# Behind the attention loop of a fused attention, Fourier mixing and MLP kernel: three engines' orders rearranged (updates in a row on POOL, weight roundings moved on ACT, the second chunk's row statistics moved on DVE)

## The reference, cut to what matters

```python
mask = q_bucket[:, :, :, None] == k_bucket[:, :, None, :]
scores = np.where(mask, scale * np.matmul(q, k.transpose(0, 1, 3, 2)), -1e9)
attn = softmax(scores)                   # 2 batches, 8 heads, 768 x 768
x = attn @ v                             # heads side by side: 2 x 768 x 512
...
X = np.fft.fft(np.fft.fft(x, axis=1), axis=2)
u = x + np.real(X)
un = (u - mean(u)) / np.sqrt(var(u) + 1e-06)        # over each row of 512
x = u + np.maximum(un @ w_ch1, 0.0) @ w_ch2         # 512 -> 2048 -> 512
...
theta = x @ w_theta
u = x + w_tok_r @ (x * cos(theta)) + w_tok_i @ (x * sin(theta))
out = u + np.maximum(u @ w_ch, 0.0)
```

## Time and profile before

| | us |
|---|---|
| median of 3 runs (780.46 to 783.19) | 782.68 |
| the profiled execution's own time | 781.82 |
| its span in the trace | 779.5 |
| PE busy | 732.8 (94%) |
| DVE busy | 438.5 (56%) |
| ACT busy | 333.8 (43%) |
| POOL busy | 298.7 (38%) |

### The profile page before, as it was taken

One profiled execution on the slowest core, in us unless ns is written; L12 is line 12 of the kernel. 1 busy time (PEld: TensorE's weight loads), 2 busy tenths in 40 slices (PEclk: granted clock), 3 DMA queues, 4 the chain that ended last, 5 costly groups with the idle time before them and its releaser, 6 DMA issues.

```text
span 779.5 us, 11008 instructions
## 1 busy us (share of the span) xinstructions
PE 732.8 (94%) x3826; PEld 615.4 (79%) x3826; DVE 438.5 (56%) x755; ACT 333.8 (43%) x693; POOL 298.7 (38%) x274
## 2 busy tenths in 40 slices
PE   3999999999998996899999999999977999999998
PEld 2788988988887775788888888888865787888876
DVE  2999999999999556623221121211146657754533
ACT  2889989988888334233101111101114333322201
POOL 3788887788784257545000000200002124312100
PEclk9999999999999997999999999999998999999999
DMA  6366644334320104322000003100012220000002
GB/s 170 96 151 149 165 103 117 95 90 116 76 72 15 42 1 135 89 74 68 1 0 1 1 1 98 51 1 0 1 55 77 62 92 27 1 14 27 14 28 81
DMA packets 48135, 47.86 MB, mean 61 GB/s; under 512 B 15828, under 2 KB 35924, under 8 KB 48084
## 3 DMA queue, kind: packets, MB, share of 16 engines
q1 hardware_dynamic: 44244, 41.65, 19.8%
q0 software_dynamic: 3840, 5.53, 2.7%
HBM read 30.26 MB, written 3.15 MB: 43 GB/s over the span
## 4 chain that ended last, share of the span: by engine, by line
PE 71%; DVE 16%; issue 5%; POOL 2%; ACT 2%; DMA 2%; SPq 1%; POOLq 0%; ACTq 0%; DVEq 0%
PE PS L908 19%; PE PS L910 19%; PE PS L909 19%; DVE negmax L1259 6%; DVE ETL L1269 4%; DVE affine L1262 2%; PE PS L999 2%; PE PS L1039 2%; PE PS L1025 2%; PE PS L1024 2%; PE PS L1040 2%; PE PS L1137 1%; PE PS L1144 1%; ACT OS L811 1%; ACT E L799 1%
## 5 line engine op out<-in xcount | busy, mean ns | idle before, releaser
L1369 DVE SCALAR_TENSOR_TENSOR HL<-PS,HH 128x512 fp32r<-128x512 f32 x48 | 33.1, 690 | 176.5 <-ACT HH L869 176.5
L869 ACT ACTIVATE HH<-PS 128x512 fp32r<-128x512 f32 x48 | 28.7, 598 | 200.2 <-PE PS L910 200.2
L799 ACT ACTIVATE E<-PS,affine 128x768 f32<-128x768 f32 x96 | 95.2, 991 | 38.3 <-DVE affine L1262 36.1
L1259 DVE TENSOR_REDUCE negmax<-PS 128x1 f32<-128x768 f32 x96 | 90.8, 945 | 16.7 <-PE PS L1025 15.5
L1269 DVE TENSOR_TENSOR ETL<-PS,ETH 128x384 fp32r<-128x384 f32 x192 | 97.1, 545 | 2.8 <-ACT ETH L792 2.8
L999 PE MATMUL PS<-ident,E 128*128 128x128 f32 x576 | 81.5, 275 | 2.3 <-DVE ETL L1269 2.3
L792 ACT ACTIVATE ETH<-PS 128x384 fp32r<-128x384 f32 x192 | 82.5, 484 | 0.9 <-PE PS L999 0.8
L908 PE MATMUL PS<-W2H,HH 128*128 128x512 f32 x192 | 75.3, 392 | 2.4 <-DVE HL L1369 2.4
L1039 PE MATMUL PS<-ETH,VHL 128*128 128x384 f32 x192 | 72.4, 377 | 5.2 <-ACT OS L811 4.6
L908 PE MATMUL PS<-UTH,W 128*128 128x512 f32 x192 | 75.8, 395 | 0.2 <-issue 0.2
L910 PE MATMUL PS<-W2H,HL 128*128 128x512 f32 x192 | 75.3, 392 | 0.0
(11 more groups left out here) (175 smaller groups left out, 1536.6 us busy)
## 6 DMA issues: line engine op xcount, KB each, us to landing
RAW<-in_moe_w_ch_dram SPq DMA_DIRECT2D x32, 256.0 KB, 2.7
QK<-in_qk_dram SPq DMA_DIRECT2D x16, 384.0 KB, 3.9
QM<-TOPH SPq DMA_DIRECT2D x16, 192.0 KB, 2.9
KM<-TOPL SPq DMA_DIRECT2D x16, 192.0 KB, 3.2
VR<-in_v_dram SPq DMA_DIRECT2D x16, 192.0 KB, 2.7
TOPL<-QM SPq DMA_DIRECT2D x16, 192.0 KB, 2.7
TOPH<-TOPH SPq DMA_DIRECT2D x16, 192.0 KB, 3.0
out_dram<-fin SPq DMA_DIRECT2D x12, 256.0 KB, 2.0
```

Of the source, the lines that this page charges most:

```text
L799: nc.scalar.activation(E[:, tile % NE, :], s_bank(tile)[:, 0:S], ACT.Exp, bias=affine[:, t, 1:2], scale=affine[:, t, 0:1], accum_out=esum[ ...
L1259: nc.vector.tensor_reduce(negmax[:, t, 1:2], s_bank(tile)[:, 0:S], AX_X, ALU.max, negate=True).then_inc(s_max, 1)
```

## The change

Four edits, none of which adds or removes an instruction of compute; SP's list of loads stays as it was.

- POOL: `update(0, 1)` stands right behind `update(0, 0)`, and `low(0)`, `low(1)` and `low(2)` are interleaved with the first two `row_scale`.
- POOL: `SCALES` becomes 18, 22, 26, 30.
- ACT: of the roundings between the `half_high` of b = 1, those of pieces 2 to 4 stay. `high(5)` moves behind `sine_part(1, 0)`, `high(6)` and `high(7)` behind `edge_part(1)`.
- DVE: `row_moments` and `normalize` of tiles 4 and 5 leave the place ahead of the MLP and go into steps 3 and 6 of its first chunk; the moments of tiles 6 to 11 go into steps 4 to 9 (they were in 3 to 8).

```diff
-SCALES = (LEAD + 1, FIRST + 10, FIRST + 14, FIRST + 18)
+SCALES = tuple(FIRST + 8 + 4 * i for i in range(4))
...
             update(0, 0)
+            update(0, 1)
+            low(0)
             row_scale(0)
-            update(0, 1)
+            low(1)
             row_scale(1)
-            low(0)
-            low(1)
+            low(2)
             update(0, 2)
-            for n in range(2, len(pieces)):
+            for n in range(3, len(pieces)):
                 low(n)
                 if n in SCALES:
                     row_scale(2 + SCALES.index(n))
...
             for g in range(TG):
                 half_high(1, g)
-                high(2 + g)
-            high(7)
+                if g < HALF:
+                    high(2 + g)
...
             sine_part(1, 0)
+            high(5)
             sine_part(1, 1)
             norm_high(2)
             norm_high(3)
             sine_part(1, 2)
             edge_part(1)
+            high(6)
+            high(7)
             high(LEAD)
             high(LEAD + 1)
...
             differences(1, 2)
-            row_moments(4)
-            row_moments(5)
-            normalize(4)
-            normalize(5)
             for c in range(NCH):
...
-                    elif c == 0 and f < HALF + QT:
-                        row_moments(QT + f - HALF)
+                    elif c == 0 and f == HALF:
+                        row_moments(4)
+                        row_moments(5)
+                    elif c == 0 and f <= HALF + QT:
+                        row_moments(QT + f - HALF - 1)
+                        if f == QT:
+                            normalize(4)
+                            normalize(5)
```

## The result

The changed kernel takes 769.79 us in the median (4 runs, 768.91 to 772.45), against 782.19 us before (4 runs): 12.4 us less, a ratio of 0.985 with a 95% interval of 0.982 to 0.988. The forecast was 769.6 us. The profiled execution took 768.91 us with a span of 766.8 us, against 781.82 and 779.5.

The account below looks back on a forecast made before the run. PE bounds the MLP, so only the two stretches ahead, where PE waits, could pay. Terms 6.7 + 2.1 + 2.6 + 1.4 + 0.35 = 13.1 us, off 782.68, gave 769.6 us; range 766.9 to 773.9.

Parts of the forecast that it names:

- POOL free at 279.4, update(0, 1) through at 281.8, low(0) at 283.0: POOL ahead of row_scale(0): its idle time would take update(0, 1) and low(0), 1.25 us, so piece 5 loads from 283.0.
- The moments of tile 2 from 284.5, the first transpose at 290.3: DVE and ACT ahead of the MLP: earlier moments and UN let PE's first transpose start at 290.3, not 296.97; 6.7 us.
- UTL at 291.55, hidden(0) at 297.4: First transpose to hidden(0): UTL at 291.55, then DVE's chain of 5.85 us, formerly 9.19 us in all; 2.1 us gained.
- shrink(0) 5.5 us behind hidden(0): hidden(0) to shrink(0): HL no longer stands behind UN, 5.5 us in place of 8.14; 2.6 us gained.
- shrink(0) and hidden(2) at 2.72 us: First MLP steps: without the idle time PE stays at full clock, 2.72 us per twelve matmuls; 1.4 + 0.35 us gained.
- What is moved at zero: Work moved into MLP steps, early high and low parts would cost nothing; transpose of tile 4 with 2.8 us spare.
- the first rival: Ahead of hidden(0): each UN waits out a whole POOL instruction, 1.8 us; gain 11.6 us, 771.1; chance 0.06.
- Rival 2: PE's clock falls between the transposes, 290.3 to 297.4, costing 1.8 to 2.4 us: 771.4 to 772; chance 0.08.
- Rival 3: shrink(0) waits for low(8) instead of HL, spare time only 0.9 us; gain 8.8 us, 773.9; chance 0.06.
- Rivals 4 and 5: 4: first stall only renamed, 779 to 783, chance 0.03; 5: UN of tile 4 late in MLP, slower, chance 0.02.

Follow-up runs that it names:

- POOL alone: Kernel before with only POOL's new order of update(0, 1) and the low parts, SCALES, ACT and DVE as before: 774.19 against 782.24 us, ratio 0.990.
- DVE alone: Kernel before with only DVE's new order (moments and UN of tiles 4 and 5 in MLP steps) and new SCALES: 779.46 against 782.24 us, 0.997.
- ACT alone: Kernel before with only ACT's new order, high(5) to high(7) moved behind: 779.56 against 782.24 us, ratio 0.997.
- the first wait filled: Kernel before plus 32 matmuls with unread result in PE's 5.7 us of idle time ahead of the first transpose: 783.19 against 782.81 us, 1.001.
- POOL and DVE: The changed kernel without ACT's edit: 772.65 against 782.24 us for the kernel before, ratio 0.989.
- low(6) twice: The changed kernel with low(6) done a second time on POOL: 772.11 against 782.81 us for the kernel before, ratio 0.987.

## Why the prediction was right, step by step

The changed kernel came to 277 us 0.34 us later than the kernel before; that is taken off the times below.

- *POOL free at 279.4, update(0, 1) through at 281.8, low(0) at 283.0*: 281.9 and 283.35. low(0) took 1.48 us, not 1.25.
- *The moments of tile 2 from 284.5, the first transpose at 290.3*: 284.6 and 290.4. **6.7 us** expected, 6.6 measured.
- *UTL at 291.55, hidden(0) at 297.4*: 291.7 and 297.4. **2.1 us**, 2.2 measured.
- *shrink(0) 5.5 us behind hidden(0)*: 5.52. **2.6 us**, 2.6 measured. low(8) ended 4.64 us behind hidden(0), where 4.6 had been put.
- *shrink(0) and hidden(2) at 2.72 us*: 2.72 each. **1.4 and 0.35 us** as put.
- *What is moved at zero*: PE was busy 256.80 of 256.80 us from hidden(2) on, with DVE at 59.71 us there, 4.8 more than before. Counted from hidden(2), row_scale(2) was through at 17.5 us (17.6 expected), the UN of tiles 4 and 5 at 27.9 (29.8), and the transpose of tile 4 came at 32.6 without a wait.

Sum 13.1, less the 0.34 us of later arrival and 0.08 us behind the MLP: the 12.7 us between the spans. The steps are confirmed one by one; that the median of 769.79 us lies only 0.2 us from the forecast is in part luck. By the medians the gain was 12.4 us and not 13.1, and the kernel before came out at 782.19 in place of the 782.68 from which the forecast was taken.

Of the rivals, the first did not come. The UN of tiles 0 and 1 took 0.54 and 1.50 us (the 1.96 in the row holds both; the prediction's 1.10, half of 2.19, was likewise 0.78 and 1.49), the next two 1.05 and 0.89. The Trainium skill ("SBUF — State Buffer", Who interferes with whom) would let a UN that takes the shared ports wait until POOL's instruction has ended, up to 1.8 us by the first rival's count. The longest here is 1.50, and it ended at 290.02, ahead of PE's first transpose (290.75), so it cost nothing. Rival 2 did not come in the changed kernel, but it did in POOL alone, with waits of 1.78 and 0.76 us, so its chance was no formality; there it cost 0.9 us and not 1.8. Its argument that PE came out of 0.80 us of waiting at full clock does not hold either: in DVE alone the clock was 0.57 behind the same wait (290.3 to 292.5). Rival 3 did not come, and its "0.9 us of spare time" was read rightly: low(8) ended 0.88 us ahead of shrink(0). Rivals 4 and 5 did not show.

What the prediction had not seen is how the parts depend on each other. It put 8.8 us on POOL's and ACT's edits together and 4.35 on DVE's. Timed, POOL alone gives 8.0, ACT alone 2.7, DVE alone 2.8; ACT's edit costs 2.5 us where DVE's is missing (8.0 down to 5.5) and goes with 2.8 more where it is there (9.6 up to 12.4, of which the trace shows 1.2 as its own). One reason is that POOL's edit and ACT's each take away the first wait by itself: with the later arrivals taken off, hidden(0) comes at 299.5 with POOL's, at 298.1 with ACT's and at 297.4 with both, from 306.2. The other is the path that all three share: high(6) to high(9), low(6) to low(9), row_scale(2), UN, HL. ACT's edit makes its start late, and DVE's takes UN and rstd off it. The change with the old SCALES was not run: row_scale(2) would stand behind low(9), waiting for moments that DVE takes in step 3, while ACT waits in step 2 for the load of piece 15, which waits for low(10) behind it. By the order of the code they would wait in a circle.

## What to carry to other kernels

When an engine waits for a tile, follow the releaser back until you meet work that does not depend on what it stands behind; here a DMA wait on ACT was caused by a buffer that POOL freed late, because POOL itself stood in a wait that an update placed behind it would have ended. On engines with one strict order, put nothing that waits for a load ahead of what the bounding engine needs next, unless its buffer has been freed at least a landing time (here 2.5 to 3.6 us) before. The mean of a row with several instructions can hide one that took three times another (UN, 0.54 and 1.50 us); read the single one where a wait depends on it. And try such edits in pairs: an edit's sign can turn with another that shares its path.

## What the runs showed of the hardware

- **The clock does not fall at every wait of the same length.** Behind 2.44 us of waiting shrink(0) took 4.14 us in the kernel before (and 4.44 in the run with the first wait filled), behind 2.24 us in POOL alone it took 2.86. Behind 0.80 us ahead of the third cosine part it stayed at 1.00 in the kernel before (289.85 to 291.20) and was 0.57 in DVE alone (290.3 to 292.5). With waits of 1.78 and 0.76 us the clock fell in POOL alone and stayed up in POOL and DVE (1.75 and 0.75). What decides it is not shown. The windows of the two, POOL alone first:

```profile
298.00:306.00 8.00, 8.00 (x34) 5.71 (x34) 4.44 (x11) 3.62 (x8) 5.60 (x6) 0.80 0.55 156
```

```profile
298.00:306.00 8.00, 7.83 (x39) 6.04 (x37) 4.89 (x8) 4.48 (x10) 6.07 (x5) 1.00 0.58 156
```

- **It can also be lower where PE never waits.** The stretch from 640 to 680 us of the run with low(6) twice, and the same stretch of the changed kernel:

```profile
640.00:680.00 40.00, 40.00 (x182) 32.98 (x181) 28.98 (x46) 11.81 (x21) 10.40 (x9) 0.96 0.00 1
```

```profile
638.50:678.50 40.00, 40.00 (x189) 33.05 (x188) 28.51 (x43) 11.58 (x19) 13.16 (x10) 1.00 0.02 7
```

  The part behind the MLP took 207.4 us in the first and 204.0 in the second, with the same instructions. Such losses are as large as the effects of single edits here, so those were read in the trace and not in the timing.
- **DVE and POOL stretch each other.** An update of X on DVE, two inputs in SBUF, took 1.77 us beside POOL's low parts (308.60) and 0.67 us beside an idle POOL (318.42 in the kernel before); a low took up to 2.34 us (305.78) against 1.25. The page of the Trainium skill named above says that a DVE instruction with two inputs in SBUF contends with POOL's reads, and these rows agree. UN shows the size of it: each UN of tiles 0 to 3 that began while a low ran ended 0.28 to 0.29 us behind the end of that low, four times in the kernel before and three times in the changed one. So it took from 0.78 to 1.50 us, depending on how much of the low was left, and 0.54 us where no low was running when it began. In the changed kernel this cost PE nothing, because PE was the bound by then; with low(6) twice the 0.4 us by which low(8) was stretched did reach it.
